# First products of a routed pair block: the slot matrix addressed by register instead of copied into a ring

## The reference

```
w = softmax(weight)                     # 8 heads, 7 taps
x[t] = sum_k w[head, k] * x[t - 6 + k]  # causal, per sequence of 3584
# soft mixture: 8 experts, 4 slots each, 32 slots in all
logits = x @ phi                        # [14336, 32]
d = softmax(logits, over tokens);  c = softmax(logits, over slots)
slots = d.T @ x                         # [32, 192]
slot_out[e] = relu(slots[e] @ w1[e]) @ w2[e]
x = c @ slot_out                        # [14336, 192]
# top-2 mixture: 8 experts, hidden width 1024
noisy = x @ w_gate + log1p(exp(x @ w_noise)) * noise
top2, gates = the two largest of noisy, softmax over them
out = sum over both: gate * relu(x @ w1[e]) @ w2[e]
```

## Time and profile before

| | |
|---|---|
| median of 3 runs | 1179.72 us (1175.39 to 1188.16) |
| the profiled execution's own time | 1186.48 us |
| its span in the trace | 1184.7 us, mean granted TensorE clock 0.922 |
| TensorE matmul | 1079.6 us, 91%, x8758 |
| VectorE | 634.8 us, 54% |
| ScalarE | 440.9 us, 37% |
| GpSimd | 325.2 us, 27% |
| L1151, high halves | x2224, 409.0 us busy, 327 ns each |
| L1155, low halves | x2224, 228.9 us busy, 246 ns each |
| L1140, first products | x2224, 171.1 us busy, 219 ns each |

### The profile page before, as it was taken

The page is one execution under the profiler, slowest core; times in us unless marked ns, Lnnn a source line. Parts: engine busy times, 40 slices in busy tenths (PEclk is TensorE's granted clock), DMA queues, the critical chain, the costliest instruction groups (busy, mean ns, idle before and its releaser), DMA issues.

```text
span 1184.7 us, 27573 instructions
## 1 busy us (share of the span) xinstructions
PE 1079.6 (91%) x8758; PEld 817.7 (69%) x8759; DVE 634.8 (54%) x1091; ACT 440.9 (37%) x818; POOL 325.2 (27%) x347
## 2 busy tenths in 40 slices
PE   6999899888884098999999999999999999999996
PEld 6999899614731022777777777777777777777774
DVE  3233523530389953556655666556556566666663
ACT  2222212110023332444444444444444444444443
POOL 4000000100003800433333333333333333333331
PEclk9999899888676555899999999999999999999998
DMA  6557755455141400333333333333333333333331
GB/s 197 172 149 233 242 191 212 134 160 163 51 124 42 186 27 0 95 111 109 111 106 110 108 110 110 100 109 110 107 106 110 108 110 110 110 106 110 109 109 41
DMA packets 76143, 142.29 MB, mean 120 GB/s; under 512 B 10876, under 2 KB 37804, under 8 KB 73800
## 3 DMA queue, kind: packets, MB, share of 16 engines
q1 hardware_dynamic: 64072, 120.72, 33.8%
q0 software_dynamic: 11120, 20.51, 5.9%
q10 hardware_dynamic: 912, 0.52, 0.2%
HBM read 67.70 MB, written 19.37 MB: 73 GB/s over the span
## 4 chain that ended last, share of the span: by engine, by line
PE 85%; DVE 6%; DMA 5%; issue 1%; another core or an unknown queue 1%; ACT 1%; POOL 0%; SPq 0%; PEldq 0%; ACTq 0%; POOLq 0%; DVEq 0%
PE ps L1151 31%; PE ps L1155 15%; PE ps L1140 10%; PE ps L946 8%; PE ps L1116 5%; DMA stage<-in_moe_w 5%; PE ps L995 3%; PE ps L997 2%; PE ps L939 2%; PE ps L1027 2%; PE ps L1095 2%; PE ps L1043 2%; PE ps L1130 1%; PE ps L1078 1%
## 5 line engine op out<-in xcount | busy, mean ns | idle before, releaser
L897 DVE SCALAR_TENSOR_TENSOR x_ring<-ps,x_ring 128x512 f16<-128x512 f32 x556 | 356.5, 682 | 277.7 <-ACT x_ring L556 159.1
L556 ACT ACTIVATE x_ring<-ps 128x512 f16<-128x512 f32 x556 | 302.3, 599 | 372.2 <-PE ps L1140 295.5
L1151 PE MATMUL ps<-w2hl,x_ring 128*128 x2224 | 409.0, 327 | 4.2 <-ACT x_ring L556 1.9
L1151 PEld LDWEIGHTS ps<-w2hl,x_ring 128*128 128x128 f16 x2224 | 207.7, 97 | 115.6 <-issue 9.1
L443 POOL DMA_INDIRECT out_rows<-x_ring,row_id x139 | 137.2, 987 | 389.7 <-DVE x_ring L906 385.5
L1155 PE MATMUL ps<-w2hl,x_ring 128*128 x2224 | 228.9, 246 | 0.0
L1155 PEld LDWEIGHTS ps<-w2hl,x_ring 128*128 128x128 f16 x2224 | 191.4, 98 | 36.6 <-DVE x_ring L897 1.8
L1140 PE MATMUL ps<-c,x_ring 96*128 96x128 f16 x2224 | 171.1, 219 | 0.0
L437 POOL DMA_INDIRECT stage<-pay_rows,row_id x139 | 134.8, 970 | 104.9 <-DVE row_id L884 62.8
L1140 PEld LDWEIGHTS ps<-c,x_ring 96*128 96x128 f16 x2224 | 140.9, 98 | 0.0
L946 PE MATMUL ps<-phi_r,xT 96*128 96x224 f32 (+6 forms) x616 | 105.7, 320 | 0.0
(11 more groups left out here) (209 smaller groups left out, 697.6 us busy)
## 6 DMA issues: line engine op xcount, KB each, us to landing
x_ring<-a SPq DMA_DIRECT2D x278, 192.0 KB
stage<-in_moe_w SPq DMA_DIRECT2D x48, 768.0 KB, 7.7
x_ring<-in_x SPq DMA_DIRECT2D x14, 1536.0 KB, 6.7
pay_rows<-x_ring SPq DMA_DIRECT2D x4, 1344.0 KB, 4.6
stage<-pay_rows,row_id POOLq DMA_INDIRECT x139, 2.5
out_rows<-x_ring,row_id POOLq DMA_INDIRECT x139
gbuf<-in_moe_noise ACTq DMA_DIRECT2D x1, 448.0 KB, 6.1
x_halo<-in_x SPq DMA_DIRECT2D x4, 72.0 KB, 3.8
```

The lines of the kernel that those rows point to most:

```text
L556: a.activation(hh[:, par, 4 * half:4 * half + 4, :].rearrange("p j q -> p (j q)"), ps[:, 2 + 2 * par + half, :], ACT.Relu).then_inc(hh_rea ...
L897: last = v.scalar_tensor_tensor(hl[:, par, 4 * half:4 * half + 4, :].rearrange("p j q -> p (j q)"), ps[:, 2 + 2 * par + half, :], 0.0, hh[ ...
L1151: t_.matmul(ps[:, 6 + b % 2, 0:2 * D], hh[:, k, j, :], w, start=k == 0 and j == 0, stop=False)
```

## The change

`first` reads its stationary operand from the tile `a3` itself, at an address that comes from the expert's number in a register. The ring `a3_blk`, the four semaphores and the sync engine's loop with its 278 copies are gone. The sync engine's wait for `a_lo`, which tells that all of `a3` is written, moves to TensorE ahead of the blocks. The number of a step is now loaded before `first` and kept for `second`; at the start of a loop pass it is loaded once more, since a register's value isn't carried into the pass.

```diff
-        a3_blk = carve(4 * F // 2)[0:KS, :].bitcast(F16).rearrange("p (a f) -> p a f", a=4)
...
-        a_in = [sem(f"a_in{i}") for i in range(4)]
...
-            sp.wait_ge(eid_ready, 1)
-            sp.wait_ge(a_lo, E)
...
-            def body(i, off, count, last):
-                for b in range(2 * off, 2 * (off + count)):
-                    m = i * (2 * BODY) + b
-                    at = slice(m, m + 1) if isinstance(m, int) else bass.ds(m, 1)
-                    e = sp.value_load(eid[0:1, at], min_val=0, max_val=E - 1)
-                    wait(sp, h_ps, m - 3)
-                    sp.dma_start(a3_blk[:, b % 4, :],
-                                 a3[:, bass.ds(e, 1), :].rearrange("p a f -> p (a f)")).then_inc(a_in[b % 4], 16)
-            block_passes(sp, body)
...
-            def first(b, k, i):
+            def first(b, k, i, e):
-                s = 2 * b + k
-                pe.wait_ge(a_in[s % 4], turns(i, s, 4, 2) * 16)
                 pe.wait_ge(c3_ready, i * BODY + (b + 1))
                 for j in range(FJ):
-                    mm = t_.matmul(ps[:, 2 + 2 * k + j // 4, (j % 4) * P:(j % 4 + 1) * P],
-                                   a3_blk[:, s % 4, j * P:(j + 1) * P], c3[:, b % 2, k, :], start=True, stop=True)
+                    rows = a3[:, bass.ds(e, 1), j * P:(j + 1) * P].rearrange("p a f -> p (a f)")
+                    mm = t_.matmul(ps[:, 2 + 2 * k + j // 4, (j % 4) * P:(j % 4 + 1) * P], rows, c3[:, b % 2, k, :],
+                                   start=True, stop=True)
                 mm.then_inc(h_ps, 1)
...
             pe.wait_ge(eid_ready, 1)
+            pe.wait_ge(a_lo, E)
             turn_c(0, 0)
             turn_c(1, 0)
-            first(0, 0, 0)
+            first(0, 0, 0, expert(0, 0, 0))
 
             def body(i, off, count, last):
...
+                e0 = expert(off, 0, i)
                 for b in range(off, off + count):
                     if not (last and b >= off + count - 2):
                         turn_c(b + 2, i)
-                    first(b, 1, i)
-                    second(b, 0, i, expert(b, 0))
+                    e1 = expert(b, 1, i)
+                    first(b, 1, i, e1)
+                    second(b, 0, i, e0)
                     if not (last and b == off + count - 1):
-                        first(b + 1, 0, i)
-                    second(b, 1, i, expert(b, 1))
+                        e0 = expert(b + 1, 0, i)
+                        first(b + 1, 0, i, e0)
+                    second(b, 1, i, e1)
```

More of the change, by code:

```diff
@@ L1157, in second, with expert @@
                 mm.then_inc(o_ps, 1)
+            def expert(b, k, i):
+                m = i * (2 * BODY) + (2 * b + k)
+                at = slice(m, m + 1) if isinstance(m, int) else bass.ds(m, 1)
+                return nc.values_load_multi_w_load_instructions(
+                    eid[0:1, at], engines=(mybir.EngineType.PE,), min_val=0, max_val=E - 1,
+                    skip_runtime_bounds_check_because="an id sums the steps of the pair starts up to a block")[1][0]
             pe.wait_ge(eid_ready, 1)
+            pe.wait_ge(a_lo, E)
             turn_c(0, 0)
             turn_c(1, 0)
-            first(0, 0, 0)
+            first(0, 0, 0, expert(0, 0, 0))
             def body(i, off, count, last):
[L1165 to L1171, removed]
+                e0 = expert(off, 0, i)
                 for b in range(off, off + count):
```

## The result

| | before | after |
|---|---|---|
| median | 1177.56 us (1175.17 to 1188.16, 4 runs) | 1278.13 us (1276.96 to 1279.34, 4 runs) |
| ratio | | 1.085, 95% interval 1.080 to 1.091 |
| span of the profiled execution | 1184.7 us | 1276.2 us |

The kernel is slower by 100.6 us. The prediction said 1255, by 75. The direction, the place and the mechanism were as forecast; the amount was a third larger.

What follows compares the result with a forecast made beforehand. TensorE's sequencer was taken to become the bound: a pass from 40.0 to 45.1 us, +76 us over 15 passes, +1 outside the loop, so +77 on the runs' median, 1256, rounded to 1255; range 1225 to 1290.

Steps and rivals of the forecast that it cites:

- The array's floor and the wait for copies: TensorE's pair blocks: array work of 39.5 us a loop pass; the dropped wait for copies costs TensorE nothing today.
- The rate of 0.124 us for a register operation with its product: TensorE's sequencer: 0.124 us each, hidden today under the array's 0.1625 us for a product with a register address.
- Rival D: First products' weight loads: a register address there is dearer, +37 to +74 us, 1292 to 1329; chance 0.06.
- The sum of a pass: TensorE's sequencer work in a loop pass: 32.4 us before, 45.1 after, so a pass goes from 40.0 to 45.1.
- the one on number loads: Loads of an expert's number on TensorE: near their 303 ns median once copies go, 0.36 us with tail, 17 a pass.
- the prediction's own figure for loads at a mean of 0.39: Number loads keeping a mean of about 0.39 us, one in four long: adds 23 us, giving 1278.
- The blocks outside the loop: 19 written-out blocks, 11 ahead and 8 behind: +0 to +0.03 us a step, +1 us for 38 steps.
- Rival A: First products: added register operations stay hidden, a pass stays at 39.5 to 40.0, time 1172 to 1180; chance 0.06.
- Rival B: Array gaps each step make the granted clock fall to 1.2 GHz in a quarter of steps, about 1405; chance 0.05.
- Rival C: Every number load is as long as the worst, 0.64 us: +87 us, about 1342; chance 0.03.
- What queues where: New waits on TensorE's sequencer: transposed pair's copy already ended; ScalarE's half comes after one whole step, with slack widened.
- The signs in the new profile: 2224 more register operations, 2.8 us steps, idle put to "issue", clock 1.00, DMA a third, loads' median near 303 ns.

Runs made afterwards that it cites:

- x2: The changed kernel with first products always reading expert 0 at a fixed address, so no register operations ahead of them and no copies: 1175.33 us, ratio 0.9986.
- x1: The kernel before, copies kept, with low-half products reading the low halves of the weights, each needing its own register operation on a moving operand: 1307 us, ratio 1.110.
- x8: The kernel before with one load for both expert numbers of a block and loop passes of 16 blocks instead of 8: 1211.12 us, ratio 1.029.
- x4: The changed kernel with first steps of a block reading the ring again (139 copies) and second steps using the register: 1212.79 us, ratio 1.029.
- x6: The changed kernel with half the steps by register, half by ring, and one load for both expert numbers of a block: 1186.79 us, ratio 1.008.
- x3: The changed kernel with the sync engine's 278 copies into the ring kept, though nobody reads them: 1331 us, ratio 1.131.
- x7: The kernel before with one load for both expert numbers of a block, nothing else changed: 1183.84 us, ratio 1.0046.

## Why the prediction was right, and where its size was off

- *The array's floor and the wait for copies.* 39.5 us a pass and no cost of the old wait: x2, with neither copies nor added register operations, runs 39.8. Right.
- *The rate of 0.124 us for a register operation with its product.* In the loop after, the distances between such operations are 0.124 at the median and 0.127 in the mean. The unknown, a register address on a weight load, costs the same as on a moving operand. Rival D had no case, and x1 shows the kind of operand to be indifferent.
- *The sum of a pass.* Taken from the starts of the sequencer's instructions between 550 and 1200 us after, 14 passes, as microseconds a pass:

```
                               predicted   measured
products (256 + 144)              32.4       33.0
number loads with their tail       6.1        7.1
bare register operations, jump     6.6        6.6
sum                               45.1       46.6
```

  The step that failed is the one on number loads: "I therefore expect the loads near their median of 303 ns". Traffic does lengthen them, as said, but I let it end with the copies. The writes of output rows still run, and in the slower step they mostly coincide with the load ahead of a second step's products: 98 such loads have a mean of 0.43 us and reach 0.52, the others have 0.30, and the mean over all loads is 0.348. That is 1.0 us a pass, 15 us in all.

  Being under way together is not enough, though: in the kernel before, the 33 loads of the loop that such writes overlapped took 0.30 us. What decides was not looked for.

  The products' 0.6 us are 9 us: operations that the row of one undisturbed stretch had at 0.124 came at 0.134 now and then. Together 24 us, and that is the difference between the 76 us forecast for the passes and the 98 measured in them (46.63 against 40.09 us, 15 times), up to rounding. The bare operations came at 0.0995 us, so the reason for rounding down to 1255 did not hold. That the prediction's own figure for loads at a mean of 0.39, 1278, is the measured time is luck: the loads gave 15 us of it and the products, for which it had nothing, 9.
- *The blocks outside the loop.* Steps of 2.53 us ahead of the loop and 2.50 behind it, worked out from the starts of first products, against 2.47 and 2.45: about +2 us where +1 was said. All that lies outside the passes lost 4.5 us: the two steps right behind the loop took 2.99 and 3.10 us, and the stage began with 7.3 us at 1.2 GHz where before it was 4.7. Right in the main: with few bare operations the sequencer nearly keeps up.
- *Rival A*, hidden register operations: x2 against the change shows that they are the loss. *Rival B*, the clock: 1.00 in the stage's trace from 472.7 to 1268.0 us, with the array streaming 85%. By the Trainium skill's page "TensorE: Matmul & The Clock Gate", section "A second HAM failure mode: psum-queue depth-cycling", a kernel with frequent small idles between its groups of matmuls had its clock swing; this trace does not agree, gaps of a few tenths of a microsecond in each step left it alone. In x8, gaps of about 3 us were followed by a fall in four cases of five. *Rival C*, long loads without the copies: partly true, by the writes of output rows: 0.52 us at most.
- *What queues where.* "The slower step widens this slack" held: no engine is named as TensorE's releaser after. The other half was missed and cost x4 its forecast: where the sequencer is ahead, that same wait caps its lead.
- *The signs in the new profile.* The operations, the step of 2.80 us, "issue" as the name of the idle time, the clock and the loads' median came as listed. The DMA share fell from 0.37 to 0.09, a quarter and not a third. The prediction's reading of the earlier trace rows passes over the last slice, which shows 6 and 8 tenths; nothing rests on it.

## What to carry to other kernels

A register address is free only while the array has more work for a product than the sequencer needs for its register operation: here 0.124 us hides behind 384 columns (0.16 us) and not behind 128 (0.055). Before an address is made dynamic, add up the sequencer's operations for a whole loop pass, number loads and jump included, and compare with the array's streaming time; a busy share of 98% says nothing about it, the count of matmuls per microsecond does. And the sum must hold between two waits that the sequencer itself stands at, not over the pass: a lead is not carried over such a wait, as far as x4 and x6 show.

## What the runs showed of the hardware

- A number load into TensorE's sequencer takes 0.30 us with no DMA traffic and up to 0.52 (the change), 0.75 (before) and 0.73 (x3) with it; two numbers in one load take 0.54 us and up to 1.04 us with traffic (x7). Traffic does not lengthen every load: in x1, with the same copies as before, the loads of the loop have a mean of 0.303 us.
- A bare register operation takes 0.09 to 0.11 us of the sequencer, one with its product 0.124, products with fixed addresses under 0.005 each: 8 of them add 0.025 us between two register operations of the trace after.
- A taken loop jump on TensorE costs 0.21 us at the median with passes of 8 blocks and 3.9 to 4.2 us with 16. The point between at which it changes was not looked for, nor was the cause shown.
- In x8 TensorE idled 2.7 to 3.3 us at each jump after a stretch in which it was busy throughout, and the granted clock then fell from 2.4 to 1.2 GHz for 3.4 us in four cases of five. The gaps of tenths of a microsecond in the change left it at 2.4 for 795 us.
